# The first expert's rows turned one phase later, and its network's products spread over the later levels

## The chip, the cores and the metric

The kernel runs on one core of a Trainium2 chip. Its time is the device time of one launch in microseconds; the time of a version is the median of its runs. TensorE does the matrix products, VectorE most of the routing, ScalarE the copies and activations, GpSimd (POOL) the indexed DMAs, and the sync engine (SP) starts the plain ones.

## What is computed

Three layers follow each other: a linear attention, a mixture of eight experts in which every token goes to exactly one expert, and a soft mixture over 32 slots. The change lies in the second.

```python
cap = N // E                        # 4352 tokens, 8 experts: 544 each
logits = x @ w_gate
order = np.argsort(-logits.flatten())
for idx in order:                   # best pairs first
    tok, e = int(idx) // E, int(idx) % E
    if assigned[tok] >= 0 or counts[e] >= cap:
        continue
    assigned[tok] = e
    counts[e] += 1
for e in range(E):
    mask = assigned == e
    out[mask] = np.maximum(x[mask] @ w1[e], 0.0) @ w2[e]
```

A row of x has 128 values, the hidden layer 1024.

## The kernel before, in words

The tokens lie as 34 tiles of 128. Behind the attention the kernel finds the experts' members in seven **phases**, one expert filled in each. A phase looks for the score at which the fullest expert reaches 544 tokens, digit by digit, in six **levels**. A level is a round trip between two engines. VectorE compares all tokens with the 32 or 64 thresholds of the digit (L1129, `thresholds`, two parts). TensorE sums them per expert (L618, 9 or 17 matmuls). VectorE copies the partial sums (L1205), TensorE folds them into counts (L628, L630), VectorE makes flags of them (L1210), TensorE sums the flags to the digit (L643), and VectorE takes the digit off and builds the next thresholds (L1220 to L1226). At the end of a phase VectorE writes the new mask (L1266), and the first L618 of the next phase waits for it.

Beside phase i the kernel does two more things. With `listing` it lists the members of the expert found in phase i-1 (`rank_members`, `list_members`, `pick_members`; VectorE writes the indices at L1108), and POOL then gathers their rows in five indexed DMAs (L371). `turn_rows` (L559 to L565) turns the gathered rows with five transposes into banks 2 and 3 of the PSUM, and ScalarE copies them to `xsT` (L826, L827). With `network` it computes the network of the expert found in phase i-2. That network is 32 **products** of two matmuls each (L524 up, L532 down), in the order up 0, up 1, down 0, up 2, down 1 and so on, each in two halves of 272 tokens; ScalarE applies the ReLU between them (L834). So phase 0 has neither, phase 1 lists expert 0, and phase 2 is the first with a network, that of expert 0.

TensorE works strictly in the order in which the code issues. The products are dealt out by hand into the places where it would wait for VectorE: `fill(count)` issues the next `count` products. Before, every phase with a network issues FIRST (2) ahead of its first L618, then in each level one while the partial sums are copied, one while the flags are made, and 4, 3, 2, 4, 3 or 2 while the digit is taken off; together 32. Behind the last level come the ties (L649 to L653), `turn_rows(i - 1)`, and `outputs(i - 2)` (L546 to L557). A phase with `listing` alone, phase 1, ends with `turn_rows(0)`.

The first product of a network waits for its weights and for `xst_copied`, the copied rows; a down product waits for its ReLU; `turn_rows` waits for its five gathers. After phase 6 the last two networks, the soft mixture and the output follow.

Of the kernel before, what the change touches and what calls it, by code (L numbers as in the profile page):

```python
# [73 lines left out]
def packing(bits):  # L74

    side = P >> bits
    return side, -(-TILES // side)


def build(nc, qT, kT, v, s12T, wg, wts, phi, u, out):  # L80
    with ExitStack() as ctx:
# [118 lines left out]
        def parts(flat, total, *sizes):  # L200
            assert sum(sizes) <= total, sizes
            at_word, views = 0, []
            for words in sizes:
# [7 lines left out]
                   for w in (w_sb, v_flat[:, 2 * CAP:2 * CAP + 2 * FF])]  # L211
# [49 lines left out]
                     for w, (a, z) in enumerate(((0, 1), (1, 5), (5, PER_QUAD))) for q in range(4)]  # L261
        OUT_BANKS = [bank for bank in OUT_BANKS if bank[2]]
        REUSED = {n: [m for m, (w1, q1, _) in enumerate(OUT_BANKS[:n]) if (w1 % 2, q1) == (w % 2, q)]
                  for n, (w, q, _) in enumerate(OUT_BANKS)}

        block = ctx.enter_context(nc.Block())
# [132 lines left out]
        def _(pe):  # L399
# [142 lines left out]
            def products(k, first, end):  # L542
                for part, f, half in PRODUCTS[first:end]:
                    part(k, f, half)

            def outputs(k):  # L546

                pe.wait_ge(S["y_copied"], k + 1)
                pe.transpose(psum[0:TAIL, 5, 0:P], yT[:, CAP - TAIL:CAP], ident[:])
                for b, rows in enumerate(rows_of):  # L550
                    mm = pe.matmul(psum[0:rows, 5, L2_COL + b * SLOTS:L2_COL + (b + 1) * SLOTS],  # L551
                                   yT[:, b * P:b * P + rows], phi_sb[:], start=True, stop=True)
                mm.then_inc(S["l2_ready"], 1)
                for b, rows in enumerate(rows_of[:-1]):
                    bank, at_col = 4, b * P
                    mm = pe.transpose(psum[0:rows, bank, at_col:at_col + P], yT[:, b * P:b * P + rows], ident[:])
                mm.then_inc(S["yt_ready"], 1)  # L557

            def turn_rows(k):  # L559

                pe.wait_ge(S["gathered"], 16 * BLOCKS * k + 16 * BLOCKS)
                for b, rows in enumerate(rows_of):
                    bank, at_col = (2, b * P) if b < BLOCKS - 1 else (3, 0)
                    mm = pe.transpose(psum[:, bank, at_col:at_col + rows], xg[0:rows, b, :], ident[0:rows, 0:rows])  # L564
                mm.then_inc(S["xt_ready"], 1)  # L565

            def rank_members(k, col):
                pe.wait_ge(S["member_ready"], k + 1)
                pe.matmul(psum[:, 1, 0:TILES], before[:], member[:, col, :], start=True, stop=True)
                pe.matmul(psum[:, 1, TILES:2 * TILES], ones_b[:], member[:, col, :], start=True, stop=True)\  # L570
                    .then_inc(S["ranks_ready"], 1)

            def list_members(k):

                pe.wait_ge(S["onehot_ready"], k + 1)
                for g in range(TILES // 2):
                    mm = pe.matmul(psum[:, 1, 0:4 * HI], onehot[:, g * P:(g + 1) * P],
                                   token_parts[:, :, :, 2 * g:2 * g + 2],
                                   start=g == 0, stop=g == TILES // 2 - 1)
                mm.then_inc(S["idx_summed"], 1)  # L580

            def pick_members(k):

                pe.wait_ge(S["listed_ready"], k + 1)
                for q in range(2):
                    for n, (w, c) in enumerate(((0, 0), (0, 1), (1, 0), (1, 1))):
                        mm = pe.matmul(psum[LO * q:LO * (q + 1), 1, LISTED:LISTED + BLOCKS],
                                       (pick2w, pick2)[w][:, c, :], listed[:, w, q:HI:2, c],
                                       start=n == 0, stop=n == 3)
                mm.then_inc(S["idx_picked"], 1)  # L590

            WHILE_COPY = [1, 1, 1, 1, 1, 1]
            WHILE_FLAGS = [1, 1, 1, 1, 1, 1]
            WHILE_DIGIT = [4, 3, 2, 4, 3, 2]
            FIRST = len(PRODUCTS) - sum(WHILE_COPY) - sum(WHILE_FLAGS) - sum(WHILE_DIGIT)

            def phase(i, listing, network):

                issued = [0]

                def fill(count):
                    if network:
                        products(i - 2, issued[0], issued[0] + count)
                        issued[0] += count

                fill(FIRST)
                pe.wait_ge(S["mask_ready"], i + 1)
                if isinstance(i, int) and i == 0:
                    pe.wait_ge(S["consts"], 6)
                for l in range(LEVELS):  # L610
                    J = 2 ** DIGITS[l]
                    side, groups = packing(DIGITS[l])
                    pick = {4: pick4, 2: pick2}[side]

                    for g in range(groups):
                        if g in (0, (groups + 1) // 2):
                            pe.wait_ge(S["above_ready"], 2 * LEVELS * i + (2 * l + (g > 0) + 1))
                        mm = pe.matmul(psum[:, 0, 0:side * EXPERTS], above[:, g * P:(g + 1) * P],  # L618
                                       mask_pad[:, :, g * side:(g + 1) * side],
                                       start=g == 0, stop=g == groups - 1)  # L620
                    mm.then_inc(S["partial_ready"], 1)
                    if listing and l == 0:
                        rank_members(i - 1, 0)
                    fill(WHILE_COPY[l])
                    if listing and l == 3:
                        pick_members(i - 1)
                    pe.wait_ge(S["partial_copied"], LEVELS * i + (l + 1))
                    pe.matmul(psum[0:J, 0, 0:EXPERTS], ones_h[:, 0:J], minus_cap[:], start=True, stop=False)  # L628
                    for c in range(side):
                        mm = pe.matmul(psum[0:J, 0, 0:EXPERTS], pick[:, c, :],  # L630
                                       partial[:, 0:side * EXPERTS].rearrange("p (e c) -> p e c", c=side)[:, :, c],
                                       start=False, stop=c == side - 1)
                    mm.then_inc(S["counts_ready"], 1)
                    if l == LEVELS - 1:
                        for d in range(LEVELS - 1):
                            pe.matmul(psum[:, 1, METS:METS + EXPERTS + 1], ones_b[0:2 ** DIGITS[d], :],
                                      flags[0:2 ** DIGITS[d], d, :], start=d == 0, stop=False)
                    fill(WHILE_FLAGS[l])
                    pe.wait_ge(S["flag_ready"], LEVELS * i + (l + 1))
                    if l == LEVELS - 1:  # L640
                        pe.matmul(psum[:, 1, METS:METS + EXPERTS + 1], ones_b[0:J, :], flags[0:J, l, :],
                                  start=False, stop=True)
                    pe.matmul(psum[:, 0, DIG:DIG + 1], sum_flags[:, l, :], flags[:, l, EXPERTS:EXPERTS + 1],  # L643
                              start=True, stop=True).then_inc(S["digit_ready"], 1)
                    fill(WHILE_DIGIT[l])
                    if listing and l == 2:
                        list_members(i - 1)
                pe.wait_ge(S["tie_ready"], i + 1)
                pe.matmul(psum[:, 1, 0:TILES], before[:], tie[:], start=True, stop=True)  # L649
                pe.matmul(psum[:, 1, TILES:2 * TILES], ones_b[:], tie[:], start=True, stop=True)\  # L650
                    .then_inc(S["tieranks_ready"], 1)
                pe.wait_ge(S["above_row_ready"], i + 1)
                pe.matmul(psum[:, 0, BASE:BASE + EXPERTS], ones_h[0:J, :], above_row[0:J, :], start=True, stop=True)\  # L653
                    .then_inc(S["base_ready"], 1)
                if listing:
                    turn_rows(i - 1)
                if network:
                    pe.wait_ge(S["y_copied"], i - 1)
                    outputs(i - 2)

            phase(0, False, False)
            phase(1, True, False)
            for i in range(2, PHASES):
                phase(i, True, True)
# [108 lines left out]
            for n in range(0, len(OUT_BANKS), 2):  # L773
# [4 lines left out]
                for step_no in range(most):  # L778
                    for w, q, tiles in pair:
                        i = step_no - (most - len(tiles))  # L780
# [638 lines left out]
```

## Time and profile before

| | |
|---|---|
| median of 3 runs | 342.2 us (341.83 to 343.26) |
| the profiled execution, its own time | 343.21 us |
| its span, first to last instruction | 341.5 us |
| TensorE, VectorE busy | 295.6 us (87%), 207.6 us (61%) |
| ScalarE, GpSimd busy | 94.0 us (28%), 87.6 us (26%) |
| mean granted TensorE clock | 0.915 of 2.4 GHz |

In the rows below, PE is TensorE's matmuls and PEld its weight loads, DVE is VectorE, ACT is ScalarE, POOL is GpSimd. L12 is a line of the kernel. A product is two matmul records, so `x4` at L524 or L532 is two products. PEclk is the clock that TensorE was granted, as a share of 2.4 GHz: 0.50 is 1.2 GHz. Times count from the first instruction. The ends of matmuls are modelled, so a full PE need not be one at its peak.

### The profile page before, as it was taken

Reading aid. Unit: us, or ns where it says so; the run is one execution under the profiler, and the core shown is the slowest. Engines: PE = TensorE matmul, PEld = TensorE weight load, DVE = VectorE, ACT = ScalarE, POOL = GpSimd, SP = SyncE. Lnnn points to the kernel's source line nnn. Section 1 sums busy time; section 2 is a strip of 40 time slices with the busy share of each in tenths; the row PEclk is TensorE's granted clock in tenths of the full one; section 3 lists DMA queues with packets and bytes.
Section 4 is the critical chain, followed back from the end, with each engine's and each line's share of the span. In section 5 each row is a group of like instructions: output and inputs, shape, how many; then the busy total and the mean of one; then the engine's idle time right before and its main releaser. Section 6 shows DMA issues by size and latency. Waiting matters only on the chain.

```text
span 341.5 us, 6748 instructions
## 1 busy us (share of the span) xinstructions
PE 295.6 (87%) x2577; PEld 226.4 (66%) x2577; DVE 207.6 (61%) x860; ACT 94.0 (28%) x200; POOL 87.6 (26%) x105
## 2 busy tenths in 40 slices
PE   6999999953334479999999999999999998999992
PEld 3789989942223257777777777777677786755471
DVE  4615287997789858787788787787864002202162
ACT  1312033420000022242251242232332534313345
POOL 5000010000000600631641551452366363302300
PEclk9999999995555559999999999999999998999998
DMA  6999702222003130122131130140142210000207
GB/s 236 404 411 422 301 2 61 63 61 77 3 0 125 32 126 2 33 53 83 33 95 41 34 132 3 33 133 7 29 131 97 65 29 12 6 2 2 65 10 261
DMA packets 15039, 31.72 MB, mean 93 GB/s; under 512 B 2848, under 2 KB 8864, under 8 KB 13984
## 3 DMA queue, kind: packets, MB, share of 16 engines
q1 hardware_dynamic: 11584, 27.46, 22.4%
q0 software_dynamic: 2560, 2.79, 3.2%
q10 hardware_dynamic: 864, 1.05, 0.9%
q8 instruction: 20, 0.33, 0.4%
q14 instruction: 11, 0.09, 0.1%
HBM read 26.28 MB, written 5.01 MB: 92 GB/s over the span
## 4 chain that ended last, share of the span: by engine, by line
PE 71%; DVE 15%; POOL 4%; issue 4%; DMA 3%; ACT 3%; ACTq 0%; SPq 0%; DVEq 0%; POOLq 0%
PE psum L524 18%; PE psum L532 17%; PE psum L419 5%; PE psum L432 5%; PE psum L618 4%; PE psum L403 3%; POOL kq_sb L371 3%; DVE feats L1129 2%; PE psum L551 2%; PE psum L697 2%; PE psum L564 2%; DVE feats L944 1%; PE psum L628 1%; DMA kq_sb<-x_by_token,tokens 1%; DVE x L1042 1%
## 5 line engine op out<-in xcount | busy, mean ns | idle before, releaser
L371 POOL DMA_INDIRECT kq_sb<-x_by_token,tokens x40 | 42.7, 1067 | 114.5 <-DVE tokens L1108 100.7
L834 ACT ACTIVATE v_flat<-psum 128x544 f32<-128x544 f32 x64 | 39.9, 624 | 101.9 <-PE psum L524 101.9
L381 POOL DMA_INDIRECT slot_logits_by_token<-kq_sb,tokens x40 | 39.0, 976 | 63.6 <-ACT kq_sb L863 53.8
L1129 DVE TENSOR_TENSOR feats<-digit_pad,steps 128x640 bf16<-128x640 int16 (+1 forms) x86 | 43.5, 539 | 0.3
L524 PE MATMUL psum<-kq_sb 128*128 128x272 f32 x128 | 39.7, 425 | 0.9 <-ACT kq_sb L827 0.9
L618 PE MATMUL psum<-mask_pad,feats 128*128 128x32 bf16 (+1 forms) x490 | 21.5, 179 | 20.9 <-DVE feats L1129 18.0
L532 PE MATMUL psum<-v_flat,kq_sb 128*128 128x272 f32 x128 | 39.2, 414 | 0.0
L524 PE MATMUL psum<-kq_sb,v_flat 128*128 128x272 f32 x128 | 38.6, 423 | 0.0
L532 PE MATMUL psum<-v_flat 128*128 128x272 f32 x128 | 37.9, 411 | 0.4 <-ACT v_flat L834 0.4
L618 PEld LDWEIGHTS psum<-mask_pad,feats 128*128 128x128 bf16 x490 | 18.7, 99 | 27.7 <-DVE feats L1129 12.8
L944 DVE TENSOR_TENSOR feats<-ab 128x2048 f32<-128x2048 f32 (+1 forms) x10 | 19.6, 1963 | 12.6 <-PE psum L432 7.6
L1324 DVE TENSOR_REDUCE cm<-vone 128x32 f32<-128x1120 f32 (+1 forms) x2 | 2.5, 1244 | 40.0 <-ACT vone L851 40.0
L524 PEld LDWEIGHTS psum<-kq_sb 128*128 128x128 f32 x128 | 22.8, 197 | 5.7 <-issue 1.4
L524 PEld LDWEIGHTS psum<-kq_sb,v_flat 128*128 128x128 f32 x128 | 23.3, 197 | 4.9 <-issue 0.2
L532 PEld LDWEIGHTS psum<-v_flat 128*128 128x128 f32 x128 | 22.3, 191 | 5.1 <-ACT v_flat L834 1.5
L532 PEld LDWEIGHTS psum<-v_flat,kq_sb 128*128 128x128 f32 x128 | 21.8, 190 | 3.7 <-ACT v_flat L834 0.2
L419 PE MATMUL psum<-wab,kq_sb 128*128 128x64 f32 x136 | 20.0, 310 | 0.9 <-DMA wab<-s12T 0.9
L419 PEld LDWEIGHTS psum<-wab,kq_sb 128*128 128x128 f32 x136 | 19.2, 225 | 2.0 <-DMA wab<-s12T 1.8
L826 ACT COPY kq_sb<-psum 128x512 f32<-128x512 f32 x8 | 4.7, 586 | 53.2 <-PE psum L564 53.2
L403 PE MATMUL psum<-warm,ones_b 128*128 128x512 bf16 x51 | 16.5, 470 | 1.7 <-DVE ones_b L923 1.7
L495 PE MATMUL psum<-kvz,featsT 128*128 128x82 f32 (+1 forms) x144 | 17.4, 269 | 0.4 <-DVE kvz L963 0.4
L495 PEld LDWEIGHTS psum<-kvz,featsT 128*128 128x128 f32 (+1 forms) x144 | 16.3, 185 | 0.8 <-ACT featsT L821 0.4
(233 smaller groups left out, 462.9 us busy)
## 6 DMA issues: line engine op xcount, KB each, us to landing
u_sb<-u SPq DMA_DIRECT2D x8, 1024.0 KB, 19.3
kq_sb<-wts SPq DMA_DIRECT2D x8, 512.0 KB, 4.5
v_flat<-wts SPq DMA_DIRECT2D x8, 512.0 KB, 4.7
kq_sb<-kT SPq DMA_DIRECT2D x4, 512.0 KB, 5.9
v_flat<-v SPq DMA_DIRECT2D x4, 512.0 KB, 6.7
kq_sb<-qT SPq DMA_DIRECT2D x4, 512.0 KB, 8.9
x_by_token<-x SPq DMA_DIRECT2D x4, 512.0 KB, 3.2
out<-x SPq DMA_DIRECT2D x4, 256.0 KB, 2.3
```

What stands on the lines that cost most here:

```text
L371: pool.indirect_dma_start(out=xg[0:rows, b, :], out_offset=None, in_=x_dram, in_offset=bass.IndirectOffsetOnAxis(ap=tokens[0:rows, which, ...
L381: pool.indirect_dma_start(out=l2_dram, out_offset=bass.IndirectOffsetOnAxis(ap=tokens[0:rows, which, b:b + 1], axis=0), in_=l2_now[0:rows, ...
L403: pe.matmul(psum[:, bank, 0:width], ones_b[:], warm[:, 0:width], start=True, stop=True)
L419: mm = pe.matmul(psum[:, n % 2, j * 64:(j + 1) * 64], src[:, t * P:(t + 1) * P], wab[:], start=True, stop=True)
L432: mm = pe.matmul(psum[:, 2 + 2 * (b % 2) + hp, 0:2 * HV], feats[a:z, g % 2, j, hp * P:(hp + 1) * P], vone[a:z, t, 2 * hp:2 * hp + 2, :], s ...
L495: mm = pe.matmul(psum[a:z, 4 + u % 4, (2 * k + hp) * NUMW:(2 * k + hp + 1) * NUMW], featsT[:, u % 2, k, hp, a:z], kvz[:, 2 * b + hp, :], s ...
L524: mm = pe.matmul(psum[:, 2 + 2 * (f % 2) + half, 0:HALF], weights[k % 2][:, f // HALF_CHUNKS, f % HALF_CHUNKS], xsT[:, half * HALF:(half + ...
L532: mm = pe.matmul(psum[:, 6 + half, 0:HALF], weights[k % 2][:, f // HALF_CHUNKS, HALF_CHUNKS + f % HALF_CHUNKS], hT[:, f % 2, half * HALF:( ...
L618: mm = pe.matmul(psum[:, 0, 0:side * EXPERTS], above[:, g * P:(g + 1) * P], mask_pad[:, :, g * side:(g + 1) * side], start=g == 0, stop=g ...
L834: act.activation(hT[:, f % 2].rearrange("p (b t) -> p b t", b=2), psum[:, 2 + 2 * (f % 2):4 + 2 * (f % 2), 0:HALF], ACT.Relu)\
L944: dve.tensor_tensor(feats[:, n % 2, 0:k].rearrange("p t (h i j) -> p (t h) i j", i=R, j=R), a, b, ALU.mult).then_inc(S["feats_ready"], 1)
L1129: dve.tensor_tensor(above[:, a * P:z * P].rearrange("p (g j c) -> p g j c", j=shape[2], c=side), digit_pad[:, a * side:z * side].rearrange ...
```

## The change

In phase 2 alone, the products ahead of the first L618 and the three fills of level 0 are left out (none, where there were 2, 1, 1 and 4), and the counts of the fills behind the digit become 0, 5, 4, 6, 4, 3. The fills of one in levels 1 to 5 stay, so all 32 products lie in levels 1 to 5. The rows of expert 0 are turned in phase 2, behind the digit matmul (L643) of level 0, instead of at the end of phase 1. All other phases issue what they issued.

```diff
@@ -592,18 +592,22 @@
             WHILE_DIGIT = [4, 3, 2, 4, 3, 2]
+            FIRST_DIGIT = [0, 5, 4, 6, 4, 3]
             FIRST = len(PRODUCTS) - sum(WHILE_COPY) - sum(WHILE_FLAGS) - sum(WHILE_DIGIT)
 
             def phase(i, listing, network):
 
                 issued = [0]
+
+                first_network = network and i == 2
...
-                fill(FIRST)
+                if not first_network:
+                    fill(FIRST)
                 pe.wait_ge(S["mask_ready"], i + 1)
...
                     if listing and l == 0:
                         rank_members(i - 1, 0)
-                    fill(WHILE_COPY[l])
+                    if l or not first_network:
+                        fill(WHILE_COPY[l])
...
-                    fill(WHILE_FLAGS[l])
+                    if l or not first_network:
+                        fill(WHILE_FLAGS[l])
                     pe.wait_ge(S["flag_ready"], LEVELS * i + (l + 1))
...
-                    fill(WHILE_DIGIT[l])
+                    if first_network and l == 0:
+                        turn_rows(0)
+                    fill((FIRST_DIGIT if first_network else WHILE_DIGIT)[l])
...
-                if listing:
+                if network:
                     turn_rows(i - 1)
```

## Rows read from the trace of the kernel before

**Rows 1.** The page: busy time of the two leading engines, clock in 40 slices.

```profile
PE 295.6 (87%) x2577; PEld 226.4 (66%) x2577; DVE 207.6 (61%) x860; ACT 94.0 (28%) x200; POOL 87.6 (26%) x105
...
PEclk9999999995555559999999999999999998999998
```

**Rows 2.** Busy time by stage, from mask to mask: phases 1, 2, 3, 4.

```profile
core 0: us, PE busy (x) PEld busy (x) DVE busy (x) ACT busy (x) POOL busy (x), PEclk, DMA share, GB/s
99.84:121.26 21.42, 9.91 (x142) 7.26 (x142) 18.95 (x93) 0.00 (x0) 5.73 (x5) 0.50 0.21 63
121.26:148.84 27.58, 26.67 (x226) 19.39 (x225) 19.55 (x94) 7.40 (x17) 5.26 (x5) 0.90 0.15 50
148.84:173.40 24.56, 24.54 (x225) 18.18 (x224) 19.70 (x95) 7.59 (x19) 10.18 (x10) 1.00 0.19 58
173.40:197.96 24.56, 24.54 (x224) 18.18 (x224) 19.67 (x95) 7.60 (x19) 10.19 (x10) 1.00 0.20 59
```

**Rows 3.** Chain of waits, end of phase 1 into phase 2 (start, us, what).

```profile
118.00 2.34 DMA kq_sb<-x_by_token,tokens
120.34 0.04 issue
120.39 1.37 PE psum L564 x5
...
121.83 0.59 ACT kq_sb L826
...
122.65 2.15 PE psum L524 x4
124.80 0.24 PE psum L618 x9
```

**Rows 4.** Timeline, phase 1, levels 0 and 1 (start, us, engine, line).

```profile
99.84 0.30 DVE L1266 TENSOR_TENSOR mask_pad<-rankx,label 128x272 bf16<-128x272 bf16 x1
...
101.96 0.19 PE L643 MATMUL psum<-flags,sum_flags 128*128 128x1 bf16 x1 [0.26 <-DVE flags L1210]
...
103.51 0.41 PE L618 MATMUL psum<-mask_pad,feats 128*128 128x16 bf16 x9 [1.37 <-DVE feats L1129]
...
104.11 0.38 PE L618 MATMUL psum<-mask_pad,feats 128*128 128x16 bf16 x8 [0.19 <-DVE feats L1129]
104.53 0.17 DVE L1205 CAST partial<-psum 128x16 f16<-128x16 f32 x1
```

**Rows 5.** Timeline, phase 2: masks 1 and 2, partial copy of level 1.

```profile
121.26 0.30 DVE L1266 TENSOR_TENSOR mask_pad<-rankx,label 128x272 bf16<-128x272 bf16 x1
...
129.62 0.17 DVE L1205 CAST partial<-psum 128x16 f16<-128x16 f32 x1 [0.31 <-PE psum L618]
...
148.84 0.30 DVE L1266 TENSOR_TENSOR mask_pad<-rankx,label 128x272 bf16<-128x272 bf16 x1
```

**Rows 6.** Busy time and clock around the two rises (columns of rows 2).

```profile
122.65:126.65 4.00, 4.00 (x23) 2.61 (x24) 0.48 (x6) 0.62 (x1) 0.00 (x0) 0.50 0.44 160
126.65:130.06 3.41, 3.41 (x30) 2.48 (x29) 2.94 (x13) 1.25 (x2) 0.00 (x0) 1.00 0.32 127
283.67:287.08 3.41, 2.47 (x21) 2.19 (x22) 0.00 (x0) 1.52 (x7) 0.00 (x0) 1.00 0.02 5
287.08:290.49 3.41, 3.41 (x10) 2.57 (x9) 2.28 (x2) 1.53 (x5) 2.05 (x3) 0.50 0.02 5
```

**Rows 7.** Chain of waits, phase 3, behind the digit of level 0.

```profile
151.78 1.02 PE psum L532 x4
152.81 0.92 PE psum L524 x4
```

**Rows 8.** Timeline, end of phase 2: last gather of expert 1, its turning.

```profile
143.91 0.87 POOL L371 DMA_INDIRECT kq_sb<-x_by_token,tokens  x1 [0.30 <-issue]
...
146.33 0.83 PE L564 MATMUL psum<-ident,kq_sb 128*128 128x128 f32 x5
```

**Rows 9.** Who waited for whom, phases 3 to 6 (us, times, longest).

```profile
PEld psum L628 <- DVE partial L1205: 5.7, 16, 0.4
```

**Rows 10.** Timeline, phase 2, level 4: both parts of the thresholds.

```profile
138.23 1.35 DVE L1129 TENSOR_TENSOR feats<-digit_pad,steps 128x1152 bf16<-128x1152 int16 x2
```

**Rows 11.** Chain of waits, phase 2, level 4: products, then partial sums.

```profile
139.13 0.46 PE psum L524 x2
139.59 0.42 PE psum L618 x17
```

## The prediction

> **What bounds the kernel now.** I read the page first, for which engine leads and where the clock stands. TensorE is busy 87% of the span, and the line of the granted clock shows its half level in six slices of the first half [rows 1]. The stages between one mask (L1266) and the next come next [rows 2]. Phase 1, without a network, takes 21.42 us with TensorE busy 9.91 of them and VectorE 18.95, so there VectorE's chain sets the pace. Phases 3 and 4 take 24.56 us each with TensorE busy 24.54, so with a network TensorE sets it. Phase 2, the one that is edited, has the same network and takes 27.58 us, 3.02 more than its successors, at a mean clock of 0.90.
>
> The chain of waits shows where the 3.02 us lie [rows 3]. The last gather of expert 0 lands at 120.34, TensorE turns the rows for 1.37 us, ScalarE copies them, and products start at 122.65. The first level's partial counts come only after two of them (L618 at 124.80), although mask 1 was written at 121.26 [rows 5]. A gap of about 0.9 us for the copies and a stretch at 1.2 GHz, which ends 4.0 us after the products began [rows 6], fill most of the excess.
>
> **The change, step by step.** The edit takes nothing away and adds no instruction: the same five transposes and the same 32 products (64 matmuls) run in another order on TensorE. No DMA, SP or POOL instruction moves.
>
> *Turning moved.* In phase 1 nothing of TensorE's follows the turning, and VectorE's chain to mask 1 does not wait for it, so mask 1 stays at 121.26. From there phase 1 itself is a template for a first level without products, at the same half clock [rows 4]. Its mask came at 99.84, its last matmul of level 0 (L643) at 101.96, its next L618 at 103.51 and 104.11, its partial copy of level 1 (L1205) at 104.53. Shifted by 21.42 us these become 123.38, 124.93, 125.53 and 125.95. The turning takes 1.37 us [rows 3] from about 123.5 to 124.9 and so just fits between L643 and L618, where the template has TensorE waiting for thresholds. I cost it at nothing; without that cover it costs up to its own 1.37 us. The rows landed at 120.34, so its own wait is over. ScalarE's copies then end near 125.7 (turning start to first product was 122.65 - 120.39 = 2.26 us, thus 125.7 here), about when the second L618 is through: nothing is lost there.
>
> *The lead.* Level 1's partial copy stood at 129.62 [rows 5]; it goes to 125.95. That is 3.67 us earlier.
>
> *The debt.* By 129.62 eight products had been done (2 first, 1, 1, 4). Now none has been by 125.95, and levels 1 to 5 carry 32 instead of 24. On a TensorE at 2.4 GHz that never waits, a product more costs 0.46 us (four matmuls queued behind others take 0.92 [rows 7]); eight cost 3.68 us. From level 1's copy to the next mask the phase took 148.84 - 129.62 = 19.22 us, all of it filled [rows 2, 5]. Lead and debt cancel: -3.67 + 3.68 = 0.0.
>
> *The clock.* What is left is the half clock. Before, it had ended ahead of the stretch that I compare. Now the products start at about 125.75, and no row shows how soon the clock rises after such a start. Bounds: it is up at once (0 us at half clock), or the moved work does not help at all and the stretch is twice the seen one (8 us). The nearest rows are the two rises of this trace: 4.0 us after the products began at 122.65, and 3.4 us after the fall at 287.08 with TensorE full all along [rows 6]. I take 4.0. At half clock four matmuls took 2.15 us [rows 3] against 1.02 after a pause at full clock [rows 7], so each microsecond of products at half clock loses (2.15 - 1.02) / 2.15 = 0.53 us. Some 0.4 us of the 4.0 are small matmuls that hardly change. The loss is 3.6 x 0.53 = 1.9 us; the ends are 0 and about 4 us.
>
> Against the row stands a row, and then a rule. From 283.67 to 287.08 TensorE was busy 2.47 of 3.41 us, mostly with transposes and narrow matmuls, and the clock fell behind it [rows 6]; so five transposes ahead of the products seem a poor way to raise it. The Trainium skill, TensorE: Matmul & The Clock Gate, section Part 4: PE-mode transpose, says that the full clock does not engage for transposes. The fall agrees with it, without proving it. By the rule the sum is +1.9; were transposes as good as products, it would be the first rival's +0.9.
>
> *Other covers.* The last gather of expert 1 is issued at 143.91 and its rows are turned at 146.33 [rows 8]. The later levels get 2, 2, 2, 1 and 1 products more, four of them behind the point where the gather's indices are ready (L1108), so the turning has 4 x 0.46 = 1.8 us more slack. ReLU keeps pace: where a down product follows, at least two products lie between it and its up pair. The weights of later experts wait for things that move with the phase. All phases behind are full in the same way, so a delay of mask 2 reaches the end whole.
>
> *Sum.* 0.0 + 1.9 = +1.9 us. The profiled execution took 343.21 us (span 341.5 and 1.7 around it), which gives 345.1. It lies 1.0 above the median of the runs, 342.2, whose range 341.83 to 343.26 is 1.4 wide, so the forecast is 342.2 + 1.9 = 344.1.
>
> **The rivals.**
>
> *The clock rises earlier.* The turning and the counts of level 1 might do for the clock what the first products did. Counted from 123.4, the same 4.0 us end at 127.4, and only 1.65 us of products are slow: 0.53 x 1.65 = +0.9, about 343.0. For it: TensorE would be near full from 123.4 on. Against: the fall at 287.08, and that 1.37 us of turning in the before raised nothing. 0.25.
>
> *The clock rises later.* If the gaps of levels 1 and 2, now with one product each beside half-speed waits, break the burst, the half clock could last 7 to 8 us: 342.2 + 3.8 = 346.0. Against: the burst that raised it at 126.65 contained L618 and the counts too. 0.09.
>
> *Faster: the products fit in holes.* A busy TensorE is modelled; the weight loads fill only 18.18 of 24.56 us in a phase [rows 2], and L628's weights wait for the partial copy each time, 5.7 us in 16 cases [rows 9]. If VectorE's thresholds and not the products end last in the later levels, the eight extra products cost nothing there, and the lead stays: -3.67 + 1.9 = -1.8, thus 340.4. It decides from the point where a threshold ends later than the products ahead of L618. Against: at level 4 of phase 2 VectorE ends at 138.23 + 1.35 = 139.58 [rows 10] and the products at 139.59 [rows 11]; the two are level, elsewhere the products end last, so at most a tenth of a microsecond hides. The Trainium skill, Perfetto Trace Analysis, section Identifying the Most-Contended Engine, says that matmul busy share is a poor measure and weight-load share the better one. By it TensorE would have a quarter of each phase free and 340.4 would be near. The chain without a pause speaks for the sum instead. 0.08.
>
> *No effect in sum.* That the lead is real but the clock happens to rise near 126.6, as before, gives 0.9 us of slow products, +0.5, 342.7. It is the early end of the first rival and is counted there.
>
> **How the numbers follow.** Main case 0.58, at 344.1 and on its own 343.2 to 345.0. A measurement of this kernel can tell about 0.5%, that is 1.7 us, and the main case lies just beyond that edge: six parts in ten slower (0.35), four the same (0.23). The early clock gives 0.22 same and 0.03 slower. The late clock gives 0.09 slower. The holes give 0.05 faster and 0.03 same. Together, rounded: faster 0.05, same 0.48, slower 0.47. The range leaves out the holes and most of the late clock, and reaches down over the early clock: 342.4 to 345.5.
>
> **What would show it.** Right: in the changed trace the turning starts about 2 us behind mask 1 and ends before the next L618; level 1's partial copy comes near 4.7 us behind mask 1 instead of 8.4; from there to mask 2 some 24.8 us instead of 19.2; the clock rises about 4 us behind the first product; mask 2 comes about 29.5 us behind mask 1 instead of 27.58; the phases behind keep 24.56. Wrong: TensorE waiting for ScalarE's copies or L618 waiting behind the turning; a rise of the clock within 2 us of the first product; the stretch from level 1 to mask 2 longer by clearly less than 3.7 us, which would mean holes; or any later phase that changes its length.

## The result, and the profile after

The changed kernel takes 343.93 us (median of 20 runs, 341.78 to 345.5), the kernel before 341.57 us over 20 runs beside it. The ratio is 1.0061, with a 95% interval of 1.0042 to 1.0079: slower by 2.1 us (the two medians lie 2.4 us apart). Here and below, a ratio leaves out slow runs, those more than 1.5% above the fastest run of their kernel. The profiled execution took 343.82 us, with a span of 342.1.

The page of the changed kernel, the rows that answer to [rows 1]:

```profile
PE 294.8 (86%) x2577; PEld 225.4 (66%) x2577; DVE 208.2 (61%) x860; ACT 94.0 (27%) x200; POOL 88.2 (26%) x105
...
PEclk9899999965555559999999999999989999999997
```

The same work is done. The clock's mean is 0.899 instead of 0.915, which is 69 us of the span at the half level instead of 58: the long stretch at half clock ends later behind the first product, two short falls are new (slices 2 and 30), and the one in slice 34 is gone. The stages between the masks, as in [rows 2]; the mask is now L1274:

```profile
core 0: us, PE busy (x) PEld busy (x) DVE busy (x) ACT busy (x) POOL busy (x), PEclk, DMA share, GB/s
96.84:118.25 21.41, 9.04 (x138) 6.55 (x138) 18.93 (x93) 0.00 (x0) 5.72 (x5) 0.50 0.20 63
118.25:148.55 30.30, 28.97 (x224) 21.21 (x225) 19.67 (x94) 6.96 (x13) 5.22 (x5) 0.82 0.14 45
148.55:173.35 24.80, 24.79 (x226) 18.46 (x227) 19.92 (x94) 7.95 (x20) 10.93 (x10) 1.00 0.19 58
173.35:197.97 24.62, 24.62 (x225) 18.26 (x224) 19.81 (x95) 7.68 (x19) 10.13 (x10) 1.00 0.20 58
```

Phase 1 is unchanged. Phase 2 takes 30.30 us instead of 27.58, and the next two 0.24 and 0.06 more: 3.0 us in this pair of executions. (This execution reached mask 1 three microseconds earlier than the one of before. Nothing of the edit lies ahead of it, and phase 1 is equally long, so the stages are compared and not the ends: the two spans differ by 0.6 us only.)

The timeline of the changed kernel in phase 2, levels 0 and 1, against [rows 3 to 5]:

```profile
118.25 0.30 DVE L1274 TENSOR_TENSOR mask_pad<-rankx,label 128x272 bf16<-128x272 bf16 x1
...
120.36 0.18 PE L649 MATMUL psum<-flags,sum_flags 128*128 128x1 bf16 x1 [0.26 <-DVE flags L1218]
...
120.40 1.34 PE L564 MATMUL psum<-ident,kq_sb 128*128 128x128 f32 x5
...
121.91 0.41 PE L622 MATMUL psum<-mask_pad,feats 128*128 128x16 bf16 x9 [0.17 <-DVE feats L1137]
...
122.93 0.17 DVE L1213 CAST partial<-psum 128x16 f16<-128x16 f32 x1
```

The turning lies where it was meant to, between the digit of level 0 and the next L622 (the old L618), and level 1's partial copy comes 4.68 us behind mask 1 instead of 8.36. From there the chain of waits of the changed kernel runs through TensorE without a pause, at first slowly:

```profile
122.51 0.38 PE psum L622 x8
122.89 1.11 PE psum L524 x2
...
124.25 1.21 PE psum L524 x2
125.46 0.00 PE psum L649
125.46 2.02 PE psum L524 x4
127.48 1.81 PE psum L532 x4
129.30 0.57 PE psum L524 x2
```

Two products take 2.02 us, and the next two, queued behind them, 1.81, where they take 1.02 and 0.92 at full clock [rows 7]. The busy time and clock of that stretch say when this ends:

```profile
122.74:125.99 3.25, 3.25 (x16) 1.99 (x14) 2.10 (x11) 0.49 (x1) 0.00 (x0) 0.50 0.56 223
125.99:129.40 3.41, 3.41 (x9) 2.60 (x8) 0.77 (x3) 0.75 (x2) 0.00 (x0) 0.50 0.02 5
```

The clock rises at 129.4, 6.7 us behind the first product, where it had risen 4.0 us behind it before [rows 6].

### The profile page after: what moved, and what is told of

It is laid out like the page before. It is cut to its first block, busy times and chain, and to the rows that moved or that the text cites. A ratio compares the mean times of both kernels' runs of the same rounds, so it can differ in the third digit from the quotient of the medians.

```text
span 342.1 us, 6748 instructions
## 1 busy us (share of the span) xinstructions
PE 294.8 (86%) x2577; PEld 225.4 (66%) x2577; DVE 208.2 (61%) x860; ACT 94.0 (27%) x200; POOL 88.2 (26%) x105
## 4 chain that ended last, share of the span: by engine, by line
PE 65%; DVE 19%; DMA 5%; issue 4%; POOL 4%; ACT 2%; SPq 1%; ACTq 0%; DVEq 0%; POOLq 0%
PE psum L524 18%; PE psum L532 17%; PE psum L432 5%; PE psum L419 4%; PE psum L622 4%; DVE feats L1137 4%; POOL slot_logits_by_token L381 2%; PE psum L551 2%; DMA slot_logits_by_token<-kq_sb,tokens 2%; PE psum L633 2%; PE psum L403 2%; DMA kq_sb<-kT 1%; DVE feats L952 1%; PE psum L705 1%; DVE x L1050 1%
## 5 line engine op out<-in xcount | busy, mean ns | idle before, releaser
L381 POOL DMA_INDIRECT slot_logits_by_token<-kq_sb,tokens x40 | 39.8, 994 | 65.0 <-ACT kq_sb L871 55.2
L622 PE MATMUL psum<-mask_pad,feats 128*128 128x32 bf16 (+1 forms) x490 | 21.9, 179 | 24.0 <-DVE feats L1137 18.4
L622 PEld LDWEIGHTS psum<-mask_pad,feats 128*128 128x128 bf16 x490 | 18.6, 100 | 30.6 <-DVE feats L1137 13.4
L532 PEld LDWEIGHTS psum<-v_flat,kq_sb 128*128 128x128 f32 x128 | 22.8, 194 | 4.2 <-ACT v_flat L842 0.2
L419 PE MATMUL psum<-wab,kq_sb 128*128 128x64 f32 x136 | 18.1, 288 | 0.9 <-DMA kq_sb<-kT 0.9
L419 PEld LDWEIGHTS psum<-wab,kq_sb 128*128 128x128 f32 x136 | 17.2, 203 | 2.1 <-DMA kq_sb<-kT 1.0
L1213 DVE CAST partial<-psum 128x32 f16<-128x32 f32 (+1 forms) x42 | 7.8, 185 | 15.1 <-PE psum L622 14.7
L403 PE MATMUL psum<-warm,ones_b 128*128 128x512 bf16 x51 | 15.5, 445 | 1.7 <-DVE ones_b L931 1.7
```

The lines of the kernel that those rows point to most:

```text
L381: pool.indirect_dma_start(out=l2_dram, out_offset=bass.IndirectOffsetOnAxis(ap=tokens[0:rows, which, b:b + 1], axis=0), in_=l2_now[0:rows, ...
L403: pe.matmul(psum[:, bank, 0:width], ones_b[:], warm[:, 0:width], start=True, stop=True)
L419: mm = pe.matmul(psum[:, n % 2, j * 64:(j + 1) * 64], src[:, t * P:(t + 1) * P], wab[:], start=True, stop=True)
L532: mm = pe.matmul(psum[:, 6 + half, 0:HALF], weights[k % 2][:, f // HALF_CHUNKS, HALF_CHUNKS + f % HALF_CHUNKS], hT[:, f % 2, half * HALF:( ...
```

## The experiments

They ran on three other chips. The kernel before takes 361.6 us on the first of these, 355.5 on the second and 356.4 on the third; a phase with a network takes about 27.6 us or more there instead of 24.56. So ratios are given against the kernel before on the same chip, and the main reading is a stretch of one profile: from level 1's partial copy to mask 2, which was 19.22 us before and 25.62 us after. Each edit is shown against the changed kernel unless it says otherwise.

**Products spread, rows turned at the end of phase 1.**

```diff
-                    if first_network and l == 0:
-                        turn_rows(0)
...
-                if network:
+                if listing:
                     turn_rows(i - 1)
```

> The products are spread as in the change, but the rows of expert 0 are turned at the end of phase 1 as before. Theory (lead and debt cancel, the half clock under the late products is the loss): the turning was hidden either way, so this is the change's time, ratio to the kernel before 1.006 (1.003 to 1.009), level 1's partial copy again 4.7 us behind mask 1, and phase 2 from mask to mask 29.5 to 30.5 us. Rival (the turning inside level 0 is what costs): ratio 1.000 to 1.002 and level 1's copy clearly earlier than 4.7 us.

Ratio 1.0047 (1.0000 to 1.0094). Level 1's copy comes 4.68 us behind mask 1, to the hundredth as in the changed kernel, and phase 2 takes 30.13 us. So the turning inside level 0 doesn't hold VectorE's chain up, and the rival that it costs there falls; the interval alone would not have told it. One thing stays open: here the clock rose 3.9 us behind the first product, against 6.7 us in the change, where the turning stands just ahead of the products. Whether that place delays the rise or the two executions only drew differently was not tested; the runs below show both short and long times with either place.

**Four products behind the digit of level 0**, rows turned as in the run above.

```diff
-            FIRST_DIGIT = [0, 5, 4, 6, 4, 3]
+            FIRST_DIGIT = [4, 4, 3, 5, 4, 2]
```

> As the run before, but four of the products go behind the digit of level 0 (4, 4, 3, 5, 4, 2). Theory: the products start at about 2.3 us behind mask 1 and most of the half clock is spent ahead of level 1's partial copy, which comes about 7.1 us behind mask 1 (before 8.4, change 4.7); the debt is four products, 1.8 us, so from that copy to mask 2 it takes 19.2 + 1.8 = 21.1 us plus at most 1 us; sum +0.6 us, ratio 1.002 (0.999 to 1.004). Rival (the clock plays no part, only the number of products behind level 0 costs, at 2.1 us for eight): ratio 1.003, and from level 1's copy to mask 2 it takes 19.2 + 4 x 0.72 = 22.1 us whatever the clock.

Ratio 0.9960 (0.9906 to 1.0014), copy 6.15 us behind mask 1, the stretch 22.71 us, phase 2 28.86 us. The copy came earlier than expected; the clock had risen 2.9 us behind the first product. The stretch lies above both expectations (21.1 to 22.1 us, and 22.1), but neither had counted what it holds towards its end: 3.3 us at half clock from a fall at 146.53, and a pause of 1.6 us. So it is inconclusive. The same kernel was run again on the third chip, with the kernel before and the change beside it.

> Rows turned at the end of phase 1, four products behind the digit of level 0, once more. Theory: from level 1's copy to mask 2 the base's stretch plus 4 x 0.46 = 1.8 us, no slow product behind that copy, ratio 1.000 (0.996 to 1.003), below the changed kernel. Rival (it beats the kernel before, as 0.996 in the earlier run hinted): 0.996 or less with an interval below 1.

There it is 1.0063 (1.0020 to 1.0106), and the rival that it beats the kernel before falls with the hint of 0.996; the expected 1.000 was missed too. The profile is of an execution of 363.33 us, well above the median of 359.79, and shows what such an execution can hold:

```profile
120.92:152.56 31.64, 29.24 (x214) 20.95 (x213) 19.53 (x95) 6.95 (x13) 5.42 (x5) 0.77 0.14 44
123.14:132.46 9.32, 9.32 (x40) 6.45 (x40) 5.11 (x20) 1.54 (x3) 0.00 (x0) 0.50 0.33 114
```

The same program had 2.9 us at half clock behind its first product in the execution above, on the first chip, and 9.3 us in this one, although TensorE shows no idle time in that stretch in either. Another fall, at 149.52, holds the last 3.0 us of the phase at half clock. The stretch took 24.98 us, 5.1 more than the kernel before takes on this chip (19.89, below) and not the 1.8 expected, with 7.9 us of it at half clock. So the expectation that no product behind that copy would be slow failed.

**The change with spare matmuls, two attempts.** The first puts 128x512 matmuls, whose results nobody uses, into waits of phase 1, and one into level 0 of phase 2. `keep_warm(bank, count, width)` issues `count` of them, 512 columns wide if no width is given.

```diff
+                        if first_network:
+                            keep_warm(7, 1)
...
+                    if listing and not network and l in (3, 4):
+                        keep_warm(7, 3 if l == 3 else 2)
...
+                if listing and not network:
+                    keep_warm(7, 6)
```

> The changed kernel with spare matmuls (128x512, results unused) in TensorE's idle time of phase 1 (levels 3 and 4, behind the base) and one in level 0 of phase 2, so that the clock is at 2.4 GHz when the first product starts. Theory: level 1's copy to mask 2 takes 22.9 us, lead and debt cancel, ratio to the kernel before 1.000 (0.997 to 1.002). Rival (extra products in the later levels cost in themselves, the clock does not matter): stays at 1.006.

Ratio 1.0018 (0.9968 to 1.0067), but the clock rose only 3.7 us behind the first product, so the condition of the test was not met; the stretch took 25.34 us. The second has more of them: in levels 3 to 5 of phase 1, eight behind its end, and again one in level 0 of phase 2.

> The changed kernel with many more spare matmuls in the waits of phase 1 (levels 3 to 5, eight behind the base) and one in level 0. Theory: if the clock is up before the first product, level 1's partial copy to mask 2 takes 22.9 us and the ratio is 1.000 (0.997 to 1.003); if it rises only in level 1 or 2 the stretch is longer by 0.53 us for each microsecond of products at half clock. Rival (extra products cost beyond 0.46 us each whatever the clock): at least 24.5 us in that stretch with the clock up, ratio 1.006.

Ratio 1.0182 (1.0134 to 1.0230), more than either side allowed. Busy time and clock of this kernel around level 0 tell what happened:

```profile
119.51:122.92 3.41, 3.41 (x19) 1.45 (x18) 3.10 (x19) 0.00 (x0) 0.00 (x0) 0.50 0.01 3
122.92:126.34 3.42, 2.24 (x33) 1.54 (x33) 2.94 (x16) 0.68 (x2) 0.00 (x0) 1.00 0.48 119
126.34:129.76 3.42, 3.42 (x11) 2.05 (x11) 2.56 (x11) 0.62 (x1) 0.00 (x0) 0.50 0.49 195
```

The clock was up at 122.92. Then came counts, the turning and the first half of level 1, with TensorE busy 2.24 us of 3.42, and at 126.34, with the first product just begun, it fell again for 3.4 us. The stretch took 25.08 us. By the theory's price it should be 22.9 + 0.53 x 3.4 = 24.7, plus what the chip adds. That accounts for the stretch and not for the ratio, which stands for 6.5 us; phase 2 took 29.83 us, some 2 us more than the kernel before takes on the third chip, and the rest is not explained.

**The same with level 0 filled too.** Against the second attempt:

```diff
                         turn_rows(0)
+                        keep_warm(7, 3)
...
+                    if first_network and l == 0:
+                        keep_warm(7, 1, 256)
```

> The changed kernel with spare matmuls in the waits of phase 1 (levels 3 to 5, behind the base) and in every wait of level 0 of phase 2 (one behind the member ranks, one of 256 columns behind the counts, three behind the turning). Theory: the clock is up before the first product and stays up, and the stretch from level 1's copy to mask 2 is the base's plus 3.7 us and no more; mask to mask then 27.6 to 28 us plus the chip's own. Rival (extra products cost more than 0.46 us each by themselves): the stretch stays as long as the changed kernel's although the clock is up.

> The kernel before itself, for its profile and as a null: ratio 1.000 (0.996 to 1.004), level 1's partial copy about 8.4 us behind mask 1, from it to mask 2 19.2 us plus at most 1.5 us of what this chip adds. Both theories say the same; it gives the other three their base on the same chip.

> The changed kernel itself on the same chip: ratio 1.006 (1.003 to 1.009), level 1's copy 4.7 us behind mask 1, from it to mask 2 the base's stretch plus 3.7 us of debt plus 0.53 us for each microsecond between the first product and the rise of the clock. Rival (the debt alone): the stretch does not depend on when the clock rises.

These three stand on one chip. The kernel before against itself gave 1.0011 (0.9973 to 1.0050), the change 1.0132 (1.0079 to 1.0185), above the 1.003 to 1.009 expected, and the filled version 1.0077 (1.0037 to 1.0118), which overlaps the change's interval. Phase 2 of each, kernel before first, then the change and its half-clock part, then the filled version:

```profile
119.44:147.42 27.98, 26.64 (x225) 19.24 (x225) 19.51 (x94) 7.40 (x17) 5.27 (x5) 0.92 0.16 49
120.74:124.12 3.38, 3.38 (x17) 2.12 (x17) 0.38 (x4) 0.62 (x1) 0.00 (x0) 0.50 0.47 113
```

```profile
120.84:152.19 31.35, 29.25 (x224) 21.11 (x225) 19.47 (x94) 6.95 (x13) 5.50 (x5) 0.82 0.14 44
125.33:131.94 6.61, 6.61 (x23) 4.54 (x21) 2.87 (x13) 1.25 (x2) 0.00 (x0) 0.50 0.31 119
```

```profile
120.16:148.40 28.24, 26.98 (x232) 19.15 (x231) 19.50 (x94) 6.96 (x13) 5.53 (x5) 1.00 0.16 49
```

The partial copies of level 1 that bound the stretch stand at 127.53 (before), 125.52 (change) and here, in the filled version:

```profile
124.89 0.18 DVE L1226 CAST partial<-psum 128x16 f16<-128x16 f32 x1
```

So the stretch is 147.42 - 127.53 = 19.89 us before, 26.67 us with the change, and 23.51 us with the change and the clock up throughout. The debt of eight products is 23.51 - 19.89 = 3.62 us. The other 3.16 us of the change, over 6.6 us at half clock, are the clock's: 0.48 us for each. Both figures rest on one profile of each version. The three stretches hold 0.43, 0.77 and 0.69 us in which TensorE is idle, so up to 0.3 us of the debt can be this chip's pauses. The rival that the extra products are dear in themselves falls.

**The kernel before with spare matmuls** around the turning (against the kernel before):

```diff
+                if listing and not network:
+                    keep_warm(7, 3)
                 if listing:
                     turn_rows(i - 1)
+                if listing and not network:
+                    keep_warm(7, 2)
```

with those of levels 3 and 4 as in the first attempt.

> The kernel before with spare matmuls in TensorE's idle time of phase 1 and on both sides of the turning. Theory: its own 4.0 us at half clock behind the first product go too, phase 2 takes 25.6 us from mask to mask instead of 27.6, ratio 0.994 (0.992 to 0.997), which is below both kernels. Rival (clock does not matter here): ratio 1.000, phase 2 stays 27.6 us.

> The kernel before with spare matmuls around the turning, once more, since the first time its interval held 1. Theory: ratio 0.994 (0.992 to 0.997), phase 2 25.6 us on a chip without other stalls. Rival: 1.000.

The two runs gave 0.9963 (0.9914 to 1.0013) and 1.0015 (0.9978 to 1.0052). Phase 2 did get shorter, though not to the 25.6 us expected: 26.80 and 26.51 us, with level 1's copy 6.38 and 6.69 us behind mask 1, against 27.98 and 8.09 in the profile of the kernel before on the third chip. The busy row of the second:

```profile
121.00:147.51 26.51, 26.15 (x226) 18.73 (x226) 19.51 (x95) 7.40 (x17) 5.26 (x5) 0.96 0.16 52
```

But the whole did not follow. The 1.5 us that phase 2 is shorter in the second run would make a ratio of 0.996, and its interval excludes that as it excludes the 0.994 expected: a miss.

**The first counts ahead of all products**, rows turned at the end of phase 1, without and with spare matmuls (three ahead of the turning, one behind it):

```diff
-            FIRST_DIGIT = [0, 5, 4, 6, 4, 3]
+            FIRST_DIGIT = [6, 3, 2, 4, 3, 2]
...
-                    if l or not first_network:
-                        fill(WHILE_COPY[l])
+                    fill(WHILE_COPY[l])
...
-                    if l or not first_network:
-                        fill(WHILE_FLAGS[l])
+                    fill(WHILE_FLAGS[l])
```

> Rows turned at the end of phase 1 as before, no spare matmuls, and in phase 2 the first counts ahead of all products (0 first, then 1 and 1, behind the digits 6, 3, 2, 4, 3, 2): the change's order of counts without its idle TensorE. Theory: products start at 1.4 us behind mask 1 as before, TensorE is as full as before, ratio 0.999 (0.996 to 1.002). Rival (counts ahead of products are harmful in themselves, or helpful in themselves): 1.004 or more, or 0.994 or less.

> Rows turned at the end of phase 1 as before, spare matmuls around the turning and in phase 1, and in phase 2 the first counts ahead of all products (0 first, then 1 and 1, behind the digits 6, 3, 2, 4, 3, 2). Theory (a full TensorE: only its idle time and its half clock count): the clock is up by about the first product and the products still start 1.4 us behind mask 1, so it is the kernel before less its 4 us at half clock and less 0.3 us, phase 2 25.3 us on a chip without other stalls, ratio 0.993 (0.990 to 0.997). Rival (the early counts shorten the phase by themselves): 2 us less than that, ratio 0.988.

Without spare matmuls 1.0068 (1.0038 to 1.0099), with them 1.0012 (0.9975 to 1.0050). The first is a miss: the products do start 1.37 us behind mask 1 as before, yet the clock rose only 5.9 us behind them, and phase 2 took 29.32 us. Perhaps the counts ahead thin out the first microseconds of products; with half clocks of 2.9 and 9.3 us in one program, that is not shown. With spare matmuls the clock was up ahead of the first product and phase 2 took 26.10 us, but the 0.993 expected was missed too: the whole is no shorter than the kernel before.

## Why the prediction was right, and where its working was not

The forecast was 344.1 us and 1.9 us slower; it came to 343.93 and 2.1 us slower. That the times agree within 0.2 us is in part luck: the forecast stands on the 342.2 us of three runs, and the kernel before came to 341.57 over 20, from which the same working gives 343.5.

- *The turning is hidden.* Right. It starts 2.15 us behind mask 1, where the template had about 2.2, and the run with the turning at its old place has level 1's copy at the same 4.68 us.
- *The lead, 3.67 us.* Right: 8.36 - 4.68 = 3.68 us.
- *The debt, 8 x 0.46 = 3.68 us.* Right: 3.62 us on one chip with the clock up. The rival of the holes falls with it. The Trainium skill, Perfetto Trace Analysis, section Identifying the Most-Contended Engine, judges TensorE's room by two measures, one of them the share of weight loads, and here that one misleads: in phase 2 of the filled version weight loads fill 19.15 of 28.24 us, and the eight products still cost their full price.
- *The half clock, 4.0 us and 1.9.* The mechanism was right and its length off. In both profiles of the change it lasted 6.6 to 6.7 us. The price, set at 0.53 us for each, measured 0.48, and 2.7 / 6.7 = 0.41 in the first pair: the stretch took 25.62 us against 22.90. The 0.53 came from four matmuls behind a pause; queued ones, 1.81 us at half clock and 0.92 at full, give (1.81 - 0.92) / 1.81 = 0.49. So phase 2 came to 30.3 us and not to the 29.5 forecast. The median moved less than this pair, by 2.1 us, so in the sum a length too short and a price too high partly offset each other. In two related kernels the half clock lasted 3.7 and 3.9 us, so 4 us is not far from what an execution may see; how long it lasted in the others is not known, as one execution of each kernel was profiled there, the change's at its median and the kernel before's 1.6 us above its own.
- *Later phases keep 24.56 us.* Off by 0.24 and 0.06. TensorE stood 1.03 us behind the mask at mask 2 before (L618 at 149.87 in the chain) and 1.48 us now, so up to 0.45 us of the delay can show only behind mask 2. The sum should have been made to TensorE's end and not to VectorE's mask.
- *The rivals of the clock.* The early one did not occur. The late one is nearer to what both profiles show than the main case, though its price of 3.8 us was not reached by the median. The row set against the early one, the fall at 287.08, was a weaker sign than the working took it for: besides transposes and narrow matmuls, its stretch holds 0.9 us of a wait for a gather, and the last section shows that the work alone doesn't bring the fall.

```profile
284.61 0.83 PE L564 MATMUL psum<-ident,kq_sb 128*128 128x128 f32 x5 [1.14 <-DMA kq_sb<-x_by_token,tokens]
```

One thing in the working is true and yet misleading. It says that lead and debt cancel and the clock is the loss. That holds against a kernel that spends 4 us at half clock itself. With the clock up on both sides, the kernel before has level 1's copy at 6.69 us and the filled change at 4.73; the lead is then 1.96 us, the debt 3.6, and the change loses 28.24 - 26.51 = 1.7 us. (The two stand on different chips; the stretches behind the copy, 19.82 and 19.89 us in the two arrangements of before, agree.) In plain words: the first product starts 4.5 us behind mask 1 instead of 1.4, and the counts that TensorE does ahead of it make up for only a part of that. The rest of each pair is the difference in half clock, 2.7 us long here and 3.2 on the third chip. At 0.48 us each these are 1.3 and 1.6 us, and with the 1.7 they give 3.0 and 3.3, where phase 2 grew by 2.7 and 3.4.

**What stays open.** On the third chip the change costs 1.0132, 4.7 us, of which phase 2 and the next hold 3.8 us in the profiles. The filled version keeps 2.7 us over the kernel before in its median, though its phase 2 is only 0.26 us longer; its profile shows 0.6 us in phase 1, of which 0.4 also stand in the change without spare matmuls, and a fall of the clock in phase 3. And the kernel before with spare matmuls gains in phase 2 and not in sum. Where this goes was not settled. No version here was shown to beat the kernel before.

## What to carry to other kernels

Where one engine is full from some point on, what counts is when its work begins and at which clock; the order of its work behind that point was expected to be worth nothing, but the run with the first counts ahead of all products, and the same start, took 0.7% more, for a reason not shown. Work that waits for nothing should not be held back for a chain that is not the bound, and a lead won on that chain must be set against the work that is owed. Sum up the full engine to its own end, and take its clock at the start of a burst as a range of several microseconds and not as a number.

## What the runs showed of the hardware that I had not expected

The rise of the clock is a wide draw. Behind the first product of phase 2 the half clock lasted 2.9 and 9.3 us in two executions of one program, on two chips, and 3.4 to 6.7 us in the seven others in which spare matmuls had not raised it before, with TensorE shown busy all the time.

The clock also falls where TensorE is nearly always busy. At the end of a phase TensorE turns rows and computes outputs, transposes and narrow matmuls; behind mask 6 it then waits 1.16 us for VectorE. The changed kernel's stretch around mask 6, and the one behind it:

```profile
245.45:248.86 3.41, 2.25 (x19) 1.90 (x19) 3.11 (x19) 1.98 (x8) 1.01 (x1) 1.00 0.01 2
248.86:252.28 3.42, 3.42 (x9) 2.49 (x8) 3.16 (x10) 0.81 (x2) 2.55 (x3) 0.50 0.57 171
```

The kernel before did the same work there, with the same wait, and its clock did not fall behind it (first row). One phase earlier in the changed kernel there is no wait, and no fall either (second row):

```profile
245.44:248.85 3.41, 2.25 (x19) 1.89 (x19) 3.11 (x19) 1.98 (x8) 1.01 (x1) 1.00 0.01 2
...
220.88:224.29 3.41, 3.39 (x32) 2.84 (x31) 3.12 (x19) 2.60 (x9) 1.01 (x1) 1.00 0.00 0
```

So neither the transposes nor the wait bring a fall each time.

Ten of the twelve profiles of the experiments hold such a fall between mask 2 and the last mask, mostly of 3.4 us and up to three times that, in phases that differ from one to the next, and up to four in one execution; two hold none there. On those chips it stands mostly 8.5 to 10 us behind a mask, and there a pause in level 1 precedes it. In the chain of the kernel before with spare matmuls (second run) it is this line, with the stretches around it below:

```profile
181.37 1.71 another core or an unknown queue
```

```profile
180.96:184.38 3.42, 2.09 (x27) 1.47 (x24) 1.69 (x10) 0.62 (x1) 1.16 (x2) 1.00 0.26 95
184.38:187.80 3.42, 3.42 (x17) 2.27 (x16) 1.93 (x8) 0.62 (x1) 0.00 (x0) 0.50 0.00 0
```

A phase with a fall in it mostly took 1.5 to 2 us longer (with the change on the third chip 29.22 us against 27.70). The falls are a part of the spread between executions, as large as the effect that was looked for, and whether a kernel's own order of work draws them was not tested.

Chips differ by more than the change: the kernel before took 341.6, 361.6 and 355 to 356 us. On the slower ones a phase with a network took about 3 us more, and nearly every phase from 3 to 6 held a pause of 1.6 to 2.6 us like the line above, for something that the profile names only as remote or unknown.
